# Token rows scattered to a DRAM region per expert, in three rounds, instead of to one sorted list at the end

## What is computed

```
# 1. a gated linear attention with complex decay, per head
S_re, S_im = decay(a_re, a_im) * S + k v^T ;  y[t] = q[t] . S_re
# 2. a mixture of 8 experts, one expert per token (argmax), capacity 384 rows
logits = x @ w_gate ; e = argmax ; gate = softmax(logits)[e]
pos = number of earlier tokens of the same expert ; keep = pos < capacity
out = keep * gate * (relu(x @ w1[e]) @ w2[e])          # 384 -> 1024 -> 384
# 3. a dense MLP, 384 -> 2048 -> 384
g = max(h, 0) + alpha * min(h, 0) with h = out @ w_in ; result = g @ w_out
```

## Time and profile before

| | us |
|---|---|
| median of 3 runs | 550.78 (550.59 to 551.64) |
| profiled execution, its own time | 550.25 |
| its span | 548.3 |
| PE busy | 469.3 (86%) |
| DVE busy | 364.2 (66%) |
| ACT busy | 278.4 (51%) |
| POOL busy | 42.9 (8%) |

### The profile page before, as it was taken

How to read it: one execution, slowest core, us unless ns; L and a number is a source line. 1 busy time by engine, 2 the same in 40 slices (tenths; PEclk the granted TensorE clock), 3 DMA queues, 4 the chain that set the end, 5 groups by cost and what they waited for, 6 DMA issues and landing times.

```text
span 548.3 us, 10022 instructions
## 1 busy us (share of the span) xinstructions
PE 469.3 (86%) x3752; PEld 419.0 (76%) x3752; DVE 364.2 (66%) x624; ACT 278.4 (51%) x451; POOL 42.9 (8%) x48
## 2 busy tenths in 40 slices
PE   0529986998997019999999999999999999999995
PEld 0327764876886019999999998898998899989985
DVE  2587798678533407767777776787757877477751
ACT  6998658764436006665666664333324333333212
POOL 2000000000001782000000000000003000020002
PEclk9968999899998558999999999999999999999999
DMA  8970000000000358676666666223224333230001
GB/s 319 422 295 2 1 2 0 3 1 2 2 2 2 140 182 321 182 215 200 203 195 202 183 197 208 85 90 115 87 86 145 90 113 101 73 117 0 1 0 60
DMA packets 22179, 63.69 MB, mean 116 GB/s; under 512 B 2929, under 2 KB 4465, under 8 KB 22129
## 3 DMA queue, kind: packets, MB, share of 16 engines
q1 hardware_dynamic: 20592, 58.27, 32.9%
q0 software_dynamic: 1536, 4.74, 2.3%
HBM read 58.27 MB, written 4.74 MB: 115 GB/s over the span
## 4 chain that ended last, share of the span: by engine, by line
PE 73%; DVE 9%; DMA 5%; issue 5%; POOL 3%; ACT 2%; SPq 2%; DVEq 0%; POOLq 0%; ACTq 0%
PE banks L1146 15%; PE banks L1144 15%; PE banks L1145 15%; PE banks L1154 7%; DMA vv<-v_rows 4%; PE banks L1155 3%; PE banks L992 3%; POOL rows_by_slot L370 3%; PE banks L980 2%; PE banks L983 2%; PE banks L944 2%; PE banks L1011 2%; PE banks L1014 1%; PE banks L1138 1%; PE banks L1040 1%
## 5 line engine op out<-in xcount | busy, mean ns | idle before, releaser
L864 DVE TENSOR_TENSOR w_lo<-raw_early,w_hi 128x768 fp32r<-128x768 f32 x84 | 80.0, 956 | 30.7 <-ACT w_hi L537 29.7
L582 ACT ACTIVATE g_hi<-g_all 128x512 fp32r<-128x512 f32 x48 | 30.3, 632 | 118.7 <-DVE g_all L917 118.7
L537 ACT ACTIVATE w_hi<-raw_early 128x768 fp32r<-128x768 f32 x84 | 70.4, 843 | 33.2 <-PE banks L1155 32.9
L1144 PE MATMUL banks<-w_hi,g_hi 128*128 128x384 f32 x192 | 65.1, 339 | 0.5 <-DVE g_lo L919 0.5
L1146 PE MATMUL banks<-w_hi,g_lo 128*128 128x384 f32 x192 | 65.1, 339 | 0.0
L1145 PE MATMUL banks<-w_lo,g_hi 128*128 128x384 f32 x192 | 64.9, 338 | 0.0
L1154 PE MATMUL banks<-h_hi_lo,w_hi 128*128 128x448 f32 x192 | 64.0, 378 | 0.9 <-DVE h_hi_lo L880 0.7
L919 DVE TENSOR_TENSOR g_lo<-g_all,g_hi 128x512 fp32r<-128x512 f32 x48 | 33.3, 693 | 44.2 <-ACT g_hi L582 44.2
L1144 PE MATMUL banks<-ys_hi,w_hi 128*128 128x512 f32 x144 | 56.1, 389 | 1.2 <-DVE ys_lo L894 1.2
L1146 PE MATMUL banks<-ys_hi,w_lo 128*128 128x512 f32 x144 | 57.1, 397 | 0.0
L1145 PE MATMUL banks<-ys_lo,w_hi 128*128 128x512 f32 x144 | 56.8, 394 | 0.0
(11 more groups left out here) (171 smaller groups left out, 992.1 us busy)
## 6 DMA issues: line engine op xcount, KB each, us to landing
raw_early<-weights SPq DMA_DIRECT2D x84, 384.0 KB, 3.6
raw_late<-weights SPq DMA_DIRECT2D x28, 384.0 KB, 3.5
xq<-q_rows SPq DMA_DIRECT2D x3, 776.0 KB, 16.2
xq<-rows_by_slot SPq DMA_DIRECT2D x12, 194.0 KB, 4.2
kk<-k_rows SPq DMA_DIRECT2D x3, 768.0 KB, 17.6
vv<-v_rows SPq DMA_DIRECT2D x3, 768.0 KB, 18.9
aa<-a_re_rows SPq DMA_DIRECT2D x2, 768.0 KB, 10.4
th<-a_im_rows SPq DMA_DIRECT2D x2, 768.0 KB, 11.7
```

The lines of the kernel that those rows point to most:

```text
L537: A(wh[:, slot, :], raw[slot], ACT.Copy).then_inc(w_hi, 1)
L582: A(gh[:, c % GBUF, :], gg[:, c % GBUF, :], ACT.Copy).then_inc(g_hi, 1)
L864: TT(wl[:, slot, :], raw[slot], wh[:, slot, :].bitcast(F32), ALU.subtract).then_inc(w_lo, 1)
L1144: MM(o, lhsT=whi, rhs=mhi, start=first, stop=False)
```

## The change

- An x row has 384 columns (XW is gone). The DRAM target has a region of 1536 rows per expert. Batch 0's tokens go downward from the middle of the region and batch 1's upward, so the two batches need not wait for each other's counts.
- `before[n]` holds, per expert and batch, the next row at block n; DVE carries it forward (`choose`), PE adds the rank within the tile (`rank`), DVE picks the token's row (`place`). This is done in three rounds: tiles 0 to 7, tiles 8 and 9, tiles 10 and 11. The first two stand in the last frame's `attend`, the third behind it. POOL scatters a round's tiles when its rows are known.
- The gate's transposes and logits move to other steps (`X_IN`, `LOGITS_IN`).
- The middle 768 rows of each region are zeroed, by eight DMAs from a zeroed part of `w0`. They stand in SP's queue behind the six weight chunks and ahead of the waits that count up `qkv_here`.
- Each expert's window of 384 rows is loaded on its own: window 0 tile by tile, windows 1 and 2 behind it, window e + 2 among the weight chunks of expert e, from window 4 on behind a wait for the end of an earlier expert. Two tiles of a window are transposed and split; those of expert e + 1 stand among the blocks of expert e (`NEXT_FROM`, `NEXT_AT`), through bank 7 alone. The third tile is for experts with more than 224 rows only. The outputs rotate over four banks.
- Gate weight and token number go through their own small DRAM list (12 more indirect DMAs), loaded back once.
- Three of the first six weight splits stand ahead of window 0, three behind.

```diff
+        ROUNDS = ((0, NB - 2), (NB - 2, NB - 1), (NB - 1, NB))
-        YE = [[bank[HID + (KB * e + d) % (8 - HID)] for d in range(KB)] for e in range(E)]
+        YE = [[bank[HID + (KB * e + d) % (7 - HID)] for d in range(KB)] for e in range(E)]
...
-        LOGITS_AT = {2: (0, 1), 3: (2, 3), 4: (4, 5), 5: (6, 7), 6: (8,), 8: (9,), 9: (10,), 10: (11,)}
+        X_IN = {2: ((0,), (1,), (2,)), 3: ((3,), (4,), (5,)), 4: ((6,), (7,), ()), 5: ((), (), (8,)),
+                7: ((9,), (), ()), 8: ((), (), (10,)), 10: ((11,), (), ())}
+        LOGITS_IN = {2: ((), (0,), (1,)), 3: ((2,), (3,), (4,)), 4: ((5,), (6,), (7,)),
+                     6: ((8,), (), ()), 7: ((), (9,), ()), 9: ((10,), (), ())}
+        NEXT_FROM = (1, 4)
+        NEXT_AT = (3, 6)
...
             for i in range(AHEAD):
                 sp.dma_start(raw[i], w_in[i, :, :]).then_inc(w_dma[i], 16)
+            sp.wait_ge(consts, 1)
+            for e in range(E):
+                sp.dma_start(xs_dram[e * REGION + MID - CAP:e * REGION + MID + CAP, :].rearrange(
+                    "(p t) w -> p t w", t=ZT), w0[0:2 * CAP // ZT, None, 0:UW].to_broadcast([2 * CAP // ZT, ZT, UW])
+                    ).then_inc(zeroed, 16)
             for f in range(NF):
                 sp.wait_ge(qkv_dma[f], 48)
                 sp.sem_inc(qkv_here, 1)
...
+            sp.wait_ge(windows, 1)
+            start_rows = [window_row(e) for e in range(FIRST)]
+            sp.wait_ge(scattered, 16 * NT)
+            for t in range(WT):
+                sp.dma_start(win[:, 0, t, :], window_rows(start_rows[0], t, 1)[:, 0, :]).then_inc(first_dma[t], 16)
             for i in range(AHEAD, RING):
                 sp.dma_start(raw[i], w_in[i, :, :]).then_inc(w_dma[i], 16)
...
-            with sp.Fori(1, E) as e:
+            for e in range(1, E):
+                if FIRST - 1 < e + FIRST - 1 < E:
+                    sp.wait_ge(used, USED_FREE + RING * max(e + FIRST - WB, 0))
+                    load_window(e + FIRST - 1, window_row(e + FIRST - 1))
                 for i in range(RING):
                     load_chunk(RING * e + i, RING * e + (i + 1 - RING), i)
+                if e == E // 2:
+                    sp.wait_ge(meta_scattered, 16 * NT)
+                    sp.dma_start(meta[:, :, :], meta_dram.rearrange("(t p) w -> p t w", p=P)).then_inc(meta_dma, 16)
...
+            pool.wait_ge(zeroed, 16 * E)
+            for r, (n0, n1) in enumerate(ROUNDS):
+                pool.wait_ge(routed, r + 1)
+                for t in range(B * n0, B * n1):
+                    pool.indirect_dma_start(xs_dram, bass.IndirectOffsetOnAxis(ap=slots_i[:, t:t + 1], axis=0),
+                                            xq[:, t * UW:(t + 1) * UW], None).then_inc(scattered, 16)
...
                 if b == 0:
                     dve.wait_ge(hop_ready, f + 1)
+                    dve.wait_ge(zeroed, 16 * E)
...
+            def choose(r):
+                n0, n1 = ROUNDS[r]
+                T = slice(B * n0, B * n1)
+                n = B * (n1 - n0)
+                dve.wait_ge(logits_made, XT_FREE + B * n1)
+                source = LB[:, T.start * E:T.stop * E].rearrange("p (t e) -> p t e", e=E)
+                if r + 1 < len(ROUNDS):
+                    dve.tensor_copy(logit[:, T, :], source).then_inc(logits_out, 1)
...
+                then(dve.tensor_reduce(top[:, T], source, AX_X, ALU.max))
+                then(TT(rt[:, 0, T, :], source, wide(top[:, T], n), ALU.is_equal))
+                then(TT(rt[:, 0, T, :], rt[:, 0, T, :], prior[:, None, :].to_broadcast([P, n, E]), ALU.mult))
+                then(dve.tensor_reduce(best[:, T], rt[:, 0, T, :], AX_X, ALU.max))
+                TT(one_hot[:, T, :], rt[:, 0, T, :], wide(best[:, T], n), ALU.is_equal).then_inc(onehot, 1)
+                dve.wait_ge(onehot, r + 1)
+                for m in range(n0, n1):
+                    TT(before[:, m + 1, 0, :], before[:, m, 0, :], one_hot[:, B * m, :], ALU.subtract)
+                    TT(before[:, m + 1, 1, :], before[:, m, 1, :], one_hot[:, B * m + 1, :], ALU.add
+                       ).then_inc(prefixed, 1)
+                    dve.wait_ge(prefixed, m + 1)
+
+            def place(r):
...
+                dve.wait_ge(ranked, r + 1)
+                then(TT(rt[:, 0, T, :], RK[:, 0:B * (n1 - n0) * E].rearrange("p (t e) -> p t e", e=E),
+                        one_hot[:, T, :], ALU.mult))
+                then(dve.tensor_reduce(slot[:, T], rt[:, 0, T, :], AX_X, ALU.add))
+                dve.tensor_copy(slots_i[:, T], slot[:, T]).then_inc(routed, 1)
...
                     if nxt is None:
+                        if s == 5:
+                            choose(0)
+                        if s == 6:
+                            place(0)
+                        if s == 7:
+                            choose(1)
+                        if s == 8:
+                            place(1)
...
+            choose(2)
+            place(2)
...
+            TT(start_i[0:1, :], ends[0:1, 0, :], low[0:1, :], ALU.max).then_inc(windows, 1)
...
+            dve.tensor_copy(wide_i[0:1, :], wide_f[0:1, :]).then_inc(flags, 1)
...
+            for e in range(E):
+                then(TT(first[:, e + 1:e + 2], first[:, e:e + 1], count[:, e:e + 1], ALU.add))
+            TT(base_i[0:1, :], first[0:1, 0:E], wide_f[0:1, :], ALU.add).then_inc(bases, 1)
+            for i in range(FIRST):
+                split_lo(i, i)
...
+            of_token(mine, move[:, :])
+            of_token(q0, start[:, :])
+            of_token(mine_n, count[:, :])
...
+            TT(meta_src[:, :, 0], gate, keep, ALU.mult).then_inc(meta_ready, 1)
+            for t in range(NTILES):
+                window_lo(0, t)
+            for i in range(FIRST, AHEAD):
+                split_lo(i, i)
...
+            def rank(r):
...
+                MM(to, lhsT=ones[:, :], rhs=before[:, n0:n1, :, :], start=True, stop=False)
+                MM(to[:, :, 0, :], lhsT=minus_upto[:, :], rhs=hot[:, :, 0, :], start=False, stop=False)
+                MM(to[:, :, 1, :], lhsT=upto[:, :], rhs=hot[:, :, 1, :], start=False, stop=True).then_inc(ranked, 1)
...
                         output(i, n)
+                        if i in NEXT_FROM and e + 1 < E:
+                            window_T(e + 1, NEXT_FROM.index(i))
```

More of the change, by code:

```diff
@@ L94, in fused_attention_moe_mlp @@
         prior = sb("prior", [P, E])
+        minus_upto = sb("minus_upto", [P, P])
+        low = sb("lowest_start", [P, E])
         logit = sb("logit", [P, NT, E])
+        one_hot = sb("one_hot", [P, NT, E])
+        before = sb("before", [P, NB + 1, B, E])
+        rt = sb("route", [P, 3, NT, E])
+        rs = sb("route_small", [P, 10, NT])
+        ends = sb("region_ends", [P, B, E])
+        count = sb("count", [P, E])
+        start = sb("window_start", [P, E])
+        first = sb("first_slot", [P, E + 1])
+        move = sb("slot_less_start", [P, E])
+        wide_f = sb("wide", [P, E])
         slots_i = sb("slots_i", [P, NT], I32)
+        comp_i = sb("compact_i", [P, NT], I32)
+        start_i = sb("start_i", [1, E], I32)
+        wide_i = sb("wide_i", [1, E], I32)
         base_i = sb("base_i", [1, E], I32)
+        meta_src = sb("meta_src", [P, NT, 2])
+        meta = sb("meta", [P, NT, 2])
         tok_slot = sb("tok_slot", [P, NT], I32)
@@ L733, in shift_state, with then, wide @@
                 TT(w0[:, c], w0[:, c], wtmp[:, :], ALU.add).then_inc(state_out, 1)
+            steps = [0]
+            def then(ins):
+                steps[0] += 1
+                ins.then_inc(route_steps, 1)
+                dve.wait_ge(route_steps, steps[0])
+            top, best, slot, q0, mine, mine_n, keep, total, gate = (rs[:, i, :] for i in range(9))
+            def wide(ap, n=NT):
+                return ap[:, :, None].to_broadcast([P, n, E])
+            def choose(r):
[6 more added lines that the diff above has]
+                    dve.tensor_copy(logit[:, T, :], source).then_inc(logits_out, 1)
+                    dve.wait_ge(logits_out, r + 1)
+                    source = logit[:, T, :]
+                then(dve.tensor_reduce(top[:, T], source, AX_X, ALU.max))
[9 more added lines that the diff above has]
+                    dve.wait_ge(prefixed, m + 1)
@@ L822, in _ @@
-            top, total, gate, keep, rank, slot = (rs[:, i, :] for i in range(6))
-            start = top
-            then(dve.tensor_reduce(top, logit[:, :, :], AX_X, ALU.max))
-            TT(rt[:, 1, :, :], logit[:, :, :], wide(top), ALU.subtract).then_inc(less_max, 1)
-            then(TT(rt[:, 0, :, :], logit[:, :, :], wide(top), ALU.is_equal))
-            then(TT(rt[:, 0, :, :], rt[:, 0, :, :], prior[:, None, :].to_broadcast([P, NT, E]), ALU.mult))
-            then(dve.tensor_reduce(rank, rt[:, 0, :, :], AX_X, ALU.max))
@@ new lines, in _, with of_token @@
+            TT(base_i[0:1, :], first[0:1, 0:E], wide_f[0:1, :], ALU.add).then_inc(bases, 1)
+            for i in range(FIRST):
+                split_lo(i, i)
```

(19 more changed lines are left out.)

316 lines of the change are left out of this document (162 added, 154 removed).

## The result

| | before | changed |
|---|---|---|
| median of 4 runs | 550.68 us (550.51 to 551.64) | 568.95 us (568.63 to 570.2) |
| profiled execution, its span | 548.3 | 567.0 |
| PE busy | 469.3 (86%) | 470.0 (83%) |
| DVE busy | 364.2 | 377.0 |
| POOL busy | 42.9 | 53.6 |

The ratio of changed to before is 1.034, with a 95% interval of 1.0327 to 1.0353. The kernel is slower by 18.3 us; the forecast was 549.3 us, and 568.95 lies outside its range.

The account below looks back on a forecast made before the run. PE was taken to bound the kernel (busy 86%) except in a 30 us hole and at the start. Hole -16.9, experts +7.1 and start +8.3 us gave -1.5, so 549.3 us, range 541 to 562.

Parts of the forecast that it names:

- The start: Kernel start: eight zeroing issues in SP's full queue delay the signal to 37.4 us, 8.3 us late; bounds 0 and 32.
- ten transfers in flight: SP's queue at the start: 9.5 to 10.2 transfers in flight; as the limit, it puts the signal at 36.0 us.
- rival 1: Start: queue counts rows, some 80 per engine; signal 28 us late, 569 us, or 18 late, 559; chance 0.34 (0.15, 0.19).
- the law with transfers: Start: SP's queue is limited by the number of transfers, not rows; the forecast's case, 549.3 us, chance 0.50.
- The frame: Last frame: from DVE's first scaling to the end of the last logits 147.2 us instead of 144.7.
- The scatters: POOL: ten of twelve issued before the last slots are known, the last ending 6 us behind the last logits, no stall.
- The hand-over: Before the experts: DVE, not the load, releases window 0's second tile; first expert product 16.4 us behind last logits, not 37.4.
- The expert stage: Experts: fourteen tiles turned on PE cost 6.6 us, window waits 0.5; the stage takes 7.1 us more.
- The MLP: MLP and end, behind the experts: nothing changes, 0 us.

Follow-up runs that it names:

- before_short: Kernel before plus eight DMAs of 96 rows (6 per engine) ahead of the waits that count up qkv_here; 553.07 us (550.52 beside it).
- long_rows: Changed kernel with the zeroing written as rows of 3,072 B instead of 1,536 B, same bytes and eight transfers, half the rows; 560.9 us in one run.
- before_plus_zero: Kernel before plus the eight zeroing DMAs at the same place, to an unread tensor, the state shift waiting for them; 577.68 us, ratio 1.0491.
- idle_queue: Changed kernel, zeroing moved behind the three signals and behind a wait for the last of six first weight chunks; 553.61 us, run again 542.44 us.
- two_zero: Changed kernel with the zeroing as two DMAs of 3,072 rows instead of eight, an expert's region cut to 768 rows; 572.9 us, ratio 1.0387.
- before_one: Kernel before plus all 6,144 zeroing rows as one DMA, 384 rows per engine, at the same place; 551.03 us in one run (551.51 beside it).
- late_memset: Changed kernel with POOL's second clearing (ys_lo) issued behind the wait for DVE's gate weights instead of ahead of it; 568.97 us, ratio 1.0322.

## Why the prediction was wrong

**The start failed, in its size.** The forecast named the place (eight issues in a full queue, ahead of the signals) and the victim (DVE, with ACT and PE behind it), and said that every microsecond after 29.1 would be lost. It then took "ten transfers in flight" from the rows of the loads and put the signal at 37.4; it came at 55.5. With +26.5 in place of +8.3 the sum would have been 567.5. The DMAs of the start bring 8 rows to an engine, so those rows of the profile cannot tell a limit of transfers from one of rows; rival 1 said so, and its 57 us for the signal and 569 us for the kernel are nearly what was measured (55.5 and 568.95). I gave the law with transfers the larger chance without a row that preferred it. Apart from the start the change gained 7.9 us by the table, where the forecast had 9.8.

**What the queue does.** Rival 1's place and price were right, its mechanism (rows in flight fill a store, and an issue waits until its own fit) only in part. What the issues took:

| kernel | rows per engine of one DMA | first issue | each further one |
|---|---|---|---|
| before_short | 6 | 3.26 | 0.42 to 0.86 |
| long_rows | 24 (3,072 B) | 3.29 | 1.25 to 3.59 |
| changed | 48 | 3.30 | 3.02 to 4.11 |
| before_plus_zero | 48 | 3.28 | 2.41 to 5.35 |
| idle_queue (nothing ahead) | 48 | 0.73 | 0.63, then 2.06 to 4.82 |
| two_zero | 192 | 3.29 | 18.16 |
| before_one | 384 | 3.28 | none |

In the same place the first is the same whatever its own size: an issue waits for what is *ahead* of it, here the weight chunks, and returns. How much of that must be gone, the windows from the start tell (columns as in the earlier trace rows), of the changed kernel and of two_zero:

```profile
0.00:52.20 52.20, 7.49 (x16) 4.02 (x16) 12.77 (x15) 27.70 (x40) 4.57 (x25) 0.79 0.99 374
```

```profile
0.00:47.56 47.56, 8.36 (x16) 4.38 (x16) 12.87 (x15) 27.69 (x40) 4.56 (x25) 0.84 0.98 372
```

The loads ahead of the zeroing are 14.2 MB. By 52.20 us 19.5 MB had moved, so 5.3 MB or some 217 rows per engine of the zeroing, of 336 issued: 119 open, 48 of the last DMA and 71 ahead of it. At the ends of the other issues, worked out the same way, it is 66 to 98 ahead, in long_rows 88, in idle_queue 57 to 78 from its third on, in two_zero (17.7 MB moved, 142 of the first 192 rows done) only 50. So an issue returns when all but some 50 to 100 rows per engine of what is ahead of it are done, and whatever its own size. The spread is more than the reading of the rows explains; one exact store that fits all does not come out, and two_zero was 3.3 us later than 80 would give.

The Trainium skill (DMA: Bandwidth & Descriptors, Why a DMA increments its semaphore by 16 and not by 1) has DMAs of up to 65,535 descriptors per engine complete. before_one agrees so far as it goes, with 384 rows per engine landing. But I had held this against rival 1, and it was no argument: a DMA longer than the store completes, and the issue behind it waits all the same.

**The frame** was right: 146.6 us from DVE's first scaling to the end of the last logits, forecast 147.2. The two ranks took 0.78 and 0.57 us of PE where 0.5 each was forecast, and among PE's waits in that stretch is none for DVE's choose and place.

**The scatters** were right: round 0 was expected at 166.2, which with 26.5 of delay is 192.7, and began at 192.68; the last ended 5.7 us behind the last logits (forecast 6); none stalled. That DVE's splits had held the one of 4.83 us is not tested by this, for none of the twelve runs beside a split now. Two of the metadata scatters do, at 221.81 and 223.81, and took 1.69 and 1.44 us against 0.96, a much shorter hold; and before, the first scatter took 1.11 us though the splits had begun.

**The hand-over** was right in who is late (DVE, not the load, releases the second tile) and 2.9 us short in size: 19.3 us instead of 16.4. Its line of small operations was forecast to hold nothing but small operations; one was held for 4.14 us. Without it, in late_memset, the stretch is 15.4 us.

**The expert stage** was right but for a size: the first two hidden blocks at the lower clock gave the 1.6 us that were forecast, and the fourteen transposes with everything else +5.8 for +7.1. If all of that is the transposes, it is 0.41 us a tile instead of 0.47. PE waited for no window. ACT waited six times for a weight chunk, 10.3 us in all and 3.2 at most, while PE's waits for hidden rows stayed at 0.5 us or less (1.6 in all, 0.7 before). A longer one, 1.34 us, came when the experts began earlier, in late_memset.

**The MLP** is 0.9 us longer where nothing was forecast. PE is busy there for 202.3 us in both kernels; no run looked for the cause.

## What to carry to other kernels

An issue into a full queue costs what the transfers ahead of it take to drain, here down to some 50 to 100 rows per engine, so price it by the rows that each engine gets and not by the number of DMAs; a signal that other engines wait for belongs ahead of bulk issues on the same queue, or the bulk goes into one DMA. If the rows of a trace fit two laws alike because all its operations have one size, the new operation of another size decides between them, and the range has to hold both. A local gain such as late_memset's shows only when the next thing in the queue, here the weight chunks behind the windows, is ready for it.

## What the runs showed of the hardware that was not expected

- The length of an issue does not depend on its own transfer: 3.26 to 3.30 us for 6 to 384 rows per engine in the same place.
- A DVE operation on 12 columns was held for 4.14 us until POOL's clearing of 5,760 columns had ended, and took 0.17 when the clearing was moved. Its neighbours of other kinds at 213.32 and 213.53 ran in 0.17 us under the same clearing. The Trainium skill (SBUF — State Buffer, Who interferes with whom) has VectorE and GpSimd share one pair of ports, locked by one of them for a whole instruction; the two rows agree with that, and show that an operation of 12 columns can be the one that is caught.
- In the last frame PE, ACT and DVE stood still for 4 to 9 us on two occasions, without a releaser in the profile, at the same place in three kernels; the two of them that were run again ran through it. It cost 11 to 12 us in the end. The kernel before, timed beside them, did not lose time (550.79 and 551.51 us). The cause is open.
